# A fused attention and gated-MLP kernel: every engine's table of places drawn up anew

## What is computed

```
cum    = cumsum(max(s, 0))                                  # per head
scores = q k^T / 8 + min(-(cum_i - cum_j), 0), causal       # 576 x 576
attn   = softmax(scores);  x = concat_heads(attn v)         # 576 x 512
gate   = sigmoid(causal convolution of x, 5 taps per channel)
y      = (gate * (x w_val)) w_out
u, v   = halves of relu(y w_in)
z      = (u * (w_spatial norm(v) + b_spatial)) w_out2       # 576 x 512
```

## Time and profile before

| what | us |
|---|---|
| median of 3 runs (502.54 to 504.51) | 504.46 |
| the profiled execution | 504.49 |
| its span, first to last instruction | 502.5 |
| TensorE busy | 470.8 (94%) |
| VectorE busy | 349.9 (70%) |
| ScalarE busy | 333.6 (66%) |
| GpSimd busy | 242.0 (48%) |

### The profile page before, as it was taken

One profiled execution on the slowest core, in us unless ns is written; L12 is line 12 of the kernel. 1 busy time (PEld: TensorE's weight loads), 2 busy tenths in 40 slices (PEclk: granted clock), 3 DMA queues, 4 the chain that ended last, 5 costly groups with the idle time before them and its releaser, 6 DMA issues.

```text
span 502.5 us, 10130 instructions
## 1 busy us (share of the span) xinstructions
PE 470.8 (94%) x3280; PEld 440.1 (88%) x3280; DVE 349.9 (70%) x826; ACT 333.6 (66%) x884; POOL 242.0 (48%) x239
## 2 busy tenths in 40 slices
PE   2599889868999999999999999999999999999997
PEld 1487777668988999999889999999889999998997
DVE  7877778989758697767577696686587786546140
ACT  4899778966977757776686657776687475334322
POOL 4576464363698536345777255245776242104000
PEclk9999999979999999999999999999999999999999
DMA  6766545743634333453343332533333201200002
GB/s 199 214 166 157 138 103 142 190 115 81 184 85 110 80 76 85 131 144 91 89 100 93 95 74 69 155 111 97 91 100 97 71 5 47 70 3 1 0 1 95
DMA packets 46566, 49.73 MB, mean 99 GB/s; under 512 B 24817, under 2 KB 29073, under 8 KB 46514
## 3 DMA queue, kind: packets, MB, share of 16 engines
q1 hardware_dynamic: 46514, 49.09, 37.1%
HBM read 25.82 MB, written 4.95 MB: 61 GB/s over the span
## 4 chain that ended last, share of the span: by engine, by line
PE 79%; DVE 8%; issue 4%; POOL 3%; ACT 2%; DMA 2%; SPq 1%; DVEq 0%; POOLq 0%
PE mix L1042 42%; PE attn_o L1010 8%; PE turned L1001 8%; PE score L1042 4%; PE attn_o L1042 4%; PE score L980 4%; PE score L981 3%; DVE u_t L896 2%; DVE prob L859 2%; PE score L987 1%; PE score L988 1%; DMA raw<-in_k 1%; POOL k L620 1%; POOL q L618 1%; POOL x_t L639 1%
## 5 line engine op out<-in xcount | busy, mean ns | idle before, releaser
L724 ACT ACTIVATE pt_hi<-turned 128x128 fp32r<-128x128 f32 (+4 forms) x160 | 65.9, 433 | 69.6 <-PE turned L1001 69.0
L868 DVE TENSOR_TENSOR pt_lo<-turned,pt_hi 128x128 fp32r<-128x128 f32 (+4 forms) x160 | 74.5, 479 | 47.8 <-ACT pt_hi L724 46.7
L715 ACT ACTIVATE prob<-prob,neg_max 128x128 f32<-128x128 f32 (+4 forms) x160 | 95.2, 600 | 17.7 <-DVE neg_max L859 17.2
L859 DVE CUSTOM_DVE_ANT_0 prob<-score,mask_b 128x128 f32<-128x128 f32 (+4 forms) x159 | 80.5, 534 | 21.6 <-PE score L988 17.6
L1001 PE MATMUL turned<-ident,prob 128*128 128x128 f32 (+1 forms) x480 | 66.7, 270 | 15.5 <-DVE pt_lo L868 13.0
L1001 PEld LDWEIGHTS turned<-ident,prob 128*128 128x128 f32 (+1 forms) x480 | 55.7, 144 | 24.2 <-issue 16.5
L618 POOL TENSOR_TENSOR q<-raw,raw_hi 64x576 fp32r<-64x576 f32 x31 | 44.9, 1448 | 57.4 <-ACT raw_hi L694 57.4
L1010 PE MATMUL attn_o<-pt_hi,v_hl 128*128 128x256 f32 (+2 forms) x224 | 61.9, 296 | 2.2 <-DVE pt_lo L868 2.2
L434 POOL TENSOR_TENSOR act_b<-u_t,act_b 128x288 fp32r<-128x288 f32 x48 | 41.0, 862 | 45.3 <-ACT act_b L794 38.7
L896 DVE SCALAR_TENSOR_TENSOR u_t<-x_t,taps,u_t 128x576 f32<-128x576 f32 x64 | 57.3, 895 | 1.6
L1010 PE MATMUL attn_o<-pt_lo,v_hl 128*128 128x256 f32 (+2 forms) x224 | 58.0, 295 | 0.0
(11 more groups left out here) (160 smaller groups left out, 981.4 us busy)
## 6 DMA issues: line engine op xcount, KB each, us to landing
q<-raw_hi SPq DMA_DIRECT2D x62, 144.0 KB
k<-raw_hi SPq DMA_DIRECT2D x62, 144.0 KB
r_bc<-r_dram SPq DMA_DIRECT2D x32, 144.0 KB, 3.0
out<-work SPq DMA_DIRECT2D x32, 144.0 KB, 1.9
raw<-in_q SPq DMA_DIRECT2D x31, 144.0 KB, 2.8
raw<-in_k SPq DMA_DIRECT2D x31, 144.0 KB, 2.8
v_raw<-in_v SPq DMA_DIRECT2D x32, 128.0 KB, 2.2
u_t<-in_moe_w_in SPq DMA_DIRECT2D x7, 256.0 KB, 3.3
```

What stands on the lines that cost most here:

```text
L715: act.activation(prob_view(i), prob_view(i), ACT.Exp, bias=neg_max[p][0:rows[i], i:i + 1], scale=-1.0, accum_out=row_sum[p][0:rows[i], i:i ...
L724: act.activation(pt_view(pt_hi, i), turned_view((g + i) % 2, i), ACT.Copy).then_inc(pt_hi_done, 1)
L859: dve.tensor_tensor_reduce(prob_view(i), score_view(g, i), mask_b[0:rows[i], at:at + width[i]], -SCALE, -LEAST, ALU.add, ALU.min, neg_max[ ...
L868: dve.tensor_tensor(pt_view(pt_lo, i), turned_view((g + i) % 2, i), pt_view(pt_hi, i).bitcast(F32), ALU.subtract).then_inc(pt_lo_done, 1)
```

## The change

Only the numbers of the table are new, and the start and pace of the `comb_mm` steps. No function is touched: the same steps with the same waits are sorted into other queues. The diff:

```
-COMB_FROM, COMB_PACE = 7.7, 1.133
-ORDER = {'pe': {'scores': [-1.0, -1.0, 0.4, 0.4, 1.25],
-        'turn': [1.75, 1.75, 3.65, 3.65, 5.25],
-        'turn_sums': 6.2,
-        'pv_first': 5.7,
-        'pv_second': -7.25,
-        'pv_rest': -8.7,
-        'mm': {'val': [0.05], 'v': [0.2, 0.3], 'u': [0.85], 'spatial': [0.75], 'out': [1.05]}},
- 'dve': {'scores': [-1.3, -1.3, -0.5, -0.5, 1.9],
-         'turn': [2.1, 2.1, 3.5, 4.35, 4.35],
-         'invert_sums': 4.25,
-         'combine': 8.45,
-         'evict': {'val': 0.25, 'spatial': 1.0},
-         'split': {'val': 2.95, 'v': 7.9, 'spatial': 3.9},
-         'stats': 2.25,
-         'norm': 4.7,
-         'x_lo': [-1.2, 0.25, 0.25, 4.45],
-         'taps': [-12.9, -12.9, -12.9, -9.1, -9.1, -9.1, -8.8, -8.8, -7.65, -7.65, -5.1, -5.1, -5.1, 2.25, 2.25, 5.5,
-                  5.5, 7.5, 7.5, 7.5],
-         'first_taps': [-15.2, -13.05, -10.3, -10.3, -7.2, -2.9, -2.9, 2.55, 2.55, 2.55, 2.55, 2.55, 2.55, 2.55, 6.45,
-                        6.45, 6.45, 6.45, 6.45, 8.2],
-         'weights_lo': [-6.0, -0.3, -0.3, -0.3, 1.1, 1.1, 6.75, 6.75, 6.75, 11.25, 19.0, 22.8, 22.8, 22.8, 22.8, 22.8,
...
-         'bias_rows': 1.7},
- 'act': {'exp': [2.25, 2.25, 2.25, 2.4, 3.95],
-         'turn': [3.2, 3.2, 4.55, 5.45, 6.3],
-         'copy_low': 9.2,
-         'split_qk': -4.5,
-         'split_v': 2.9,
-         'x_hi': [0.25, 0.25, 1.6, 6.45],
-         'tanh': [-2.85, 5.2, 9.1, 10.8],
-         'evict': {'v': 3.0, 'u': 2.3, 'out': 2.55},
-         'keep_sums': 7.45,
-         'guard_sums': 4.85},
...
- 'pool': {'split_qk': -4.9,
-          'split_v': 3.2,
-          'divide': 9.95,
-          'stats': 4.05,
-          'split': {'val': 4.2, 'v': 7.2, 'spatial': 3.2},
...
- 'sp': {'load_qk': -10.45,
-        'place_qk': -5.5,
-        'load_v': -2.05,
-        'store_sums': 6.55,
-        'spread_sums': 8.55,
-        'evict': {'out': 1.7},
...
+COMB_FROM, COMB_PACE = 9.4, 1.043
+ORDER = {'pe': {'scores': [-1.3, -1.3, 0.4, 0.4, 2.45],
+        'turn': [1.15, 1.15, 3.5, 3.5, 5.1],
+        'turn_sums': 5.55,
+        'pv_first': 4.95,
+        'pv_second': 6.25,
+        'pv_rest': 0.4,
+        'mm': {'val': [-0.45], 'v': [-0.2, 0.55], 'u': [0.6], 'spatial': [0.85], 'out': [0.75]}},
+ 'dve': {'scores': [-1.0, -1.0, 0.4, 0.4, 2.1],
+         'turn': [1.75, 1.75, 3.8, 5.0, 5.0],
+         'invert_sums': 4.15,
+         'combine': 8.45,
+         'evict': {'val': 0.0, 'spatial': 0.85},
+         'split': {'val': 2.75, 'v': 5.75, 'spatial': 3.2},
+         'stats': 3.3,
+         'norm': 4.8,
+         'x_lo': [2.45, 2.45, 2.45, 4.0],
+         'taps': [-12.85, -12.65, -12.65, -12.65, -12.65, -8.35, -8.35, -8.35, -3.45, -3.45, -3.45, -1.6, -1.6, 1.3,
+                  1.95, 5.35, 6.3, 7.25, 7.25, 7.25],
+         'first_taps': [-17.7, -8.45, -8.45, -8.45, -7.25, -4.15, -3.3, -3.05, 1.65, 1.65, 1.65, 5.95, 5.95, 5.95,
+                        5.95, 5.95, 5.95, 6.25, 6.25, 7.25],
+         'weights_lo': [-0.25, 1.4, 1.4, 1.4, 6.85, 6.85, 8.9, 8.9, 13.5, 13.5, 18.2, 18.2, 18.2, 18.2, 19.45, 19.45,
...
+         'bias_rows': 3.7},
+ 'act': {'exp': [1.5, 1.5, 2.6, 2.6, 4.4],
+         'turn': [2.35, 2.35, 4.3, 6.4, 6.4],
+         'copy_low': 9.15,
+         'split_qk': -4.15,
+         'split_v': 2.0,
+         'x_hi': [-0.75, 2.75, 2.75, 5.7],
+         'tanh': [-2.55, 7.2, 8.15, 10.35],
+         'evict': {'v': 3.15, 'u': 2.35, 'out': 2.15},
+         'keep_sums': 7.35,
+         'guard_sums': 5.7},
...
+ 'pool': {'split_qk': -0.8,
+          'split_v': 4.75,
+          'divide': 12.8,
+          'stats': 8.7,
+          'split': {'val': 6.9, 'v': 11.0, 'spatial': 5.55},
...
+ 'sp': {'load_qk': -4.2,
+        'place_qk': -2.1,
+        'load_v': 1.6,
+        'store_sums': 10.65,
+        'spread_sums': 11.05,
+        'evict': {'out': 6.55},
...
```

36 lines of the change are left out of this document (18 added, 18 removed).

## The result

The changed kernel takes 499.88 us (median of 5 runs, 499.51 to 501.88) against 504.46 us before (also 5 runs, 502.54 to 504.72): ratio 0.9928, 95% interval 0.9913 to 0.9943, so 0.72% or some 4.6 us faster. The forecast was 495.2 us, a gain of 9.3 us. The time is in the forecast's range and the sign is right, but the gain is just under half; it is the time of the rival "gains eaten" (499.5 us). The profiled execution of the changed kernel is its slowest, 501.88 us (span 499.8 us). The spans of the two profiles differ by 2.6 us, all of it there by head 3; behind the first heads they run nearly in step. The medians lie between the two.

The account below looks back on a forecast made before the run. TensorE has 470.83 us of work in a 502.5 us span, nearly all winnable idle time before 120 us. 2.8 + 3.0 + 2.9 + 1.0 + 0.3 - 0.7 = 9.3 us less, 504.5 to 495.2 us; range 489 to 503 us.

Parts of the forecast that it names:

- gains eaten: Rival: gains overlap or are eaten by full ScalarE and VectorE; only some 5 us come, 499.5 us; chance 0.19.
- (a): Opening: less VectorE work ahead of the first low halves shortens TensorE's 3.30 us wait; 2.8 us won, ends 0 and 3.3.
- (b): Rounds of two heads, 45 to 85 us: SyncE stores and spreads sums sooner; 3.0 us won, ends 0 and 5.1.
- (c): First join: fewer taps ahead of head 7's sum, sums stored sooner; first val product 2.9 us earlier, ends 0 and 5.5.
- (d): TensorE's clock from 105 us: a shorter wait may avoid the drop; 1.0 us won, ends 0 and 2.0.
- (e): Nine instead of six taps behind the join: a 1.3 us stall replaces 1.59 us; 0.3 us won.
- (f): TensorE's order, pv_first and next transposes earlier: wins nothing while TensorE is full; uncovered, 0.3 to 1 us lost a head.
- (g): Later joins: VectorE's x_lo of group 3 ahead of the inverse and two low halves; 0.7 us lost, ends 0 and 12.
- VectorE held behind the divide: Rival: at later joins and heads 11, 19, 27 VectorE waits for spread sums, delaying low halves; 511.5 us, chance 0.09.

Follow-up runs that it names:

- second profile: The changed kernel run and profiled again, nothing edited: median 500.19 us, profiled execution 499.18 us, span 497.2 us.
- place_first: Changed kernel with SyncE's loads of weights 8 and 9 moved behind the placing of head 1 and the load of head 2: 1.6 to 2.5 us slower than it.
- place_two: Changed kernel with SyncE's loads of weights 8 to 11 put behind the placing of head 2: 1.6 to 2.5 us slower than the changed kernel.
- join_mend: Changed kernel, ScalarE's low copy of head 7 ahead of its high parts, VectorE's x_lo 0 to 2 behind head 7's sum: 1.2 to 1.5 us slower.
- sp_only: Kernel before with only SyncE's table of the changed kernel: 2.0 to 2.3 us of the gain.
- gap_fill: Changed kernel, weight parts moved behind the join, combined-weight products copied sooner and stretched: 2 us above the 504.6 us of the same without the stretch.

## Why the prediction was right or wrong

The sign, the stages in which the gain would come and two of the sizes were right. By step:

- **(a) opening, 2.8 us forecast.** The named transposes came 2.85 us sooner, but turn_sums of head 0 only 0.8 us (26.34 to 25.53 us; 1.5 us in the second profile) and of head 1 1.4 us (2.1 us). The step failed where it read "VectorE keeps two of the three low parts ahead" and stopped at VectorE: it did not follow SyncE's queue, where a load of weights waits for the first of those low parts with the placing of head 1 behind. That was so before the change too: SyncE began to place head 1 at 15.87 us before, and at 16.86 and 15.63 us in the two profiles after. In the old order TensorE's 3.30 us wait hid it. The scores of head 1 stood at 22.14 us before and now start when their keys land, at 21.31 and 20.64 us: 0.8 and 1.5 us sooner, which is all that came. `place_first` and `place_two` show one more link behind that. The third of 4.18 us for one low part was an average too: the three took 0.69 us and then 1.8 to 1.9 us each beside GpSimd.
- **(b) rounds of two heads, 3.0 us forecast.** Right in size: 2.7 us less idle time (3.5 us in the second profile), 2.5 us of it by SyncE's table alone. The reason is borne out in part: GpSimd waited 22.6 us before 120 us for the spread sums, and now 3.9 us for them and 12.1 us for VectorE's sum of the head, 5.17 us of it at head 5, where 5.43 us stood. The store of head 1's sums went at 37.55 us against the 37.44 us worked out.
- **(c) first join, 2.9 us forecast.** From turn_sums of head 7 to the first val product it was 14.5 us (93.42 to 107.94) and is 12.9 us (91.05 to 103.99): 1.6 us. The chain of the forecast (store, spread, divide, x_lo 3) did become shorter, and then was not the last to arrive: the sum of head 7, made at 99.33 us behind three taps, three x_lo and a low part of weights, came later than the spread sums (in `join_mend`, with the sum early, GpSimd did wait for the spread sums, 1.27 us). The step that failed is "the sums 2.3 us sooner", which took the divide to wait for the spread sums alone. The kernel before already showed the other arrival, in VectorE's timeline:

```profile
103.22 0.75 DVE L876 TENSOR_TENSOR x_t<-attn_o,x_t 64x576 f32<-64x576 f32 x1
```

  This sum ended at 103.97 us, 0.3 us ahead of the divide at 104.30 us, so sooner sums alone could win no more than 0.3 us; `sp_only` made them sooner and won nothing there. In the changed kernel the divide came 1.7 us sooner against turn_sums of head 7 (9.2 instead of 10.9 us behind it), with four taps fewer in front of the sum and three x_lo and a low part of weights in their place.
- **(d) clock, a gain of 1.0 us forecast.** The wrong sign, and the term that was furthest off. TensorE's busy time rose by 2.2 us in the first and 2.5 us in the second profile. The stretches in which TensorE worked at the lower level are the opening, by the durations (see the last section), and one at the join where the column reads 0.50. First the kernel before:

```profile
0.00:26.91 26.91, 11.29 (x41) 8.95 (x42) 19.80 (x42) 17.87 (x40) 14.88 (x20) 1.00 0.71 208
102.01:108.83 6.82, 4.12 (x17) 3.96 (x18) 6.64 (x17) 4.16 (x11) 4.45 (x3) 0.50 0.46 110
```

then the changed one, first and second profile:

```profile
0.00:26.98 26.98, 12.55 (x46) 10.00 (x47) 19.99 (x45) 18.49 (x43) 16.32 (x21) 1.00 0.73 210
98.66:105.48 6.82, 5.15 (x20) 4.45 (x21) 6.19 (x15) 5.80 (x16) 5.18 (x4) 0.50 0.39 93
...
0.00:26.87 26.87, 13.20 (x48) 10.41 (x49) 18.71 (x47) 18.90 (x45) 17.21 (x22) 1.00 0.77 217
98.55:105.38 6.83, 6.43 (x26) 5.40 (x25) 6.22 (x15) 4.99 (x15) 6.41 (x5) 0.50 0.42 93
```

  The slow stretch at the join is as long as before, 6.8 us. Before, TensorE's wait filled 2.7 us of it; now the wait is shorter or over when the clock falls, and more of the stretch is work: 5.15 and 6.43 us instead of 4.12 us. At the opening the same happens, because more instructions now lie before 27 us: 12.55 and 13.20 us of work instead of 11.29 us. About half of such time is lost (L1010's products start 0.21 us apart at 100.68 us and 0.12 us apart at 89.43 us, in the first profile), an estimate that gives 0.5 and 1.2 us more at the join, 0.6 and 1.0 us more at the opening, together 1.1 of the 2.2 us and 2.1 of the 2.5 us. Where the rest comes from stays open. The forecast's step was that a shorter wait costs less clock; the rows show that it gives back work to a slow stretch of the same length. The rule that I cited (the Trainium skill, TensorE: Matmul & The Clock Gate, "HAM oscillation": idle gaps bring the half clock unless they are short) would, as I read it, have kept the full clock over a gap of 2 to 3 us. The rows do not agree: the clock fell at 98.66 us, inside the 2.88 us wait (97.45 to 100.33 us), in the first profile, and at 98.55 us, 0.8 us behind the same wait, in the second. In `gap_fill` it stayed up over a wait of 0.81 us. The rule made the sum 1.0 us lower, further from the result.
- **(e) taps behind the join, 0.3 us forecast.** A wait of 1.49 us stands at 111.78 us against 1.59 us before, but only 0.33 us in the second profile, so the 0.3 us lies inside what two profiles differ by. What waits is a value product, for its eviction (L913) behind six taps, and not a transpose for its low half.
- **(f) the rest of TensorE's order, 0 forecast.** Wrong in kind. Put back alone it costs 10 us, put in alone 11 us. That TensorE is full was no reason to value its order at nothing: what it hides depends on which low halves and sums VectorE makes first. The forecast named the cover and not that VectorE's order had to change with it. The new wait for the sum of the head before belongs to this step, and it was not foreseen.
- **(g) later joins, -0.7 us forecast.** The size was right by luck and the cause wrong: 1.0 us was lost after 120 us, at 172 us, to the new wait of step (f), and nothing to x_lo. At head 23 the divide came 9.4 us behind turn_sums (320.88 less 311.51 us) against 9.7 us taken, and x_lo 3 was in time.

The idle time won by the first profile is 4.9 us and by the second 7.8 us, against 8.3 us by the steps without the clock. In the second profile it is 2.1 us in 12 to 25 us, 3.5 in 45 to 85, 2.2 in 85 to 105 and 1.2 in 105 to 120, less 1.0 behind 120 us and 0.3 in the rest: near the forecast stage by stage. The medians lie between the two profiles. The missing half, 4.7 us, is thus first the clock's step (1.0 forecast, -2.2 to -2.5 measured), and then the chains in (a) and (c) that ended at another engine's queue. One reading in the prediction was slightly off and entered no term: the last 78 us reach 0.5 us past the span, so they lose 2.7 us and not 3.2 us.

Of the rivals, "gains eaten" had the time and half of the reason (chains that share engines). "VectorE held behind the divide" did not happen. GpSimd's share of the SBUF ports, mentioned there on one stretched tap, set what moving x_lo cost at the join: the Trainium skill (GPSIMD Engine Reference, "Specifications") says that GpSimd shares its SBUF interfaces with VectorE, and the rows agree (x_lo three times in 2.11, 3.31 or 4.50 us).

## What to carry to other kernels

When the queues of five engines are written anew together, a change of one table can't be priced alone: look for what each moved instruction now stands behind on its own engine and on the engine that feeds it, and take as the gain of a chain only what is left when the second latest arrival is known. A stall that becomes shorter does not give its time back in full if the clock still falls in it, since the work that follows sooner is then done slowly. The latest arrival of a chain hides the second latest: in the trace before the change it stood only 0.3 us behind. Where VectorE and GpSimd both work, a free slot for VectorE is one in which GpSimd waits, and the place in the queue counts as much as the length.

## What the runs showed of the hardware

- Two engines slow each other: the same three VectorE instructions (128x576, fp32r from f32) took 2.11 us with GpSimd idle, 3.31 us beside one of its instructions and 4.50 us beside three; GpSimd's 1.41 us instructions took 1.90 us. Where one starts just ahead of the other it keeps its time: VectorE's low part took 0.69 us when it started 0.12 us ahead of GpSimd's instruction and 1.92 us when it started 0.04 us behind it.
- In the first 27 us the granted clock reads 1.00, but five transposes of 96x96 take 1.00 us there (at 23.14 us before and 23.18 us in the changed kernel), which is what they take at a granted clock of 0.50 (101.32 us), and 0.58 us later on. The column of the clock can't be read before that point; the durations can.
- One kernel, two profiles: 2.6 us apart, with VectorE's first low part taking 1.92 us in one and 0.69 us in the other, and ScalarE waiting 1.52 us for the load of head 4's keys in one and not at all in the other. A single timeline of this kernel carries that much on its own.
